# Scan and mixture of experts: logits formed together with the turning back of the rows, rows stored in 4 KB pieces, and another order of work at the end of the first sort

## The reference

```
# scan, for each of 2 sequences of 5056 steps, 256 features
f = lower_bound + (1 - lower_bound) * sigmoid(f_logit);  h = f*h + (1-f)*x;  y[t] = h
# layer 1: 10112 rows, 8 experts, F = 1024
logits = (y/|y|) @ (emb/|emb|).T / tau;  e = argmax(logits)
gate = softmax(logits)[e];  out = gate * (relu(y @ w1[e]) @ w2[e])
# layer 2: the same with logits = out @ w_gate and its own w1, w2
```

## Time and profile before

| | |
|---|---|
| median of 3 runs | 1317.83 us |
| profiled execution | 1315.59 us, span 1313.8 us |
| TensorE busy | 1279.0 us, 97% |
| VectorE busy | 973.1 us, 74% |
| ScalarE busy | 825.5 us, 63% |
| GpSimd busy | 430.6 us, 33% |

### The profile page before, as it was taken

The page is one execution under the profiler, slowest core; times in us unless marked ns, Lnnn a source line. Parts: engine busy times, 40 slices in busy tenths (PEclk is TensorE's granted clock), DMA queues, the critical chain, the costliest instruction groups (busy, mean ns, idle before and its releaser), DMA issues.

```text
span 1313.8 us, 30682 instructions
## 1 busy us (share of the span) xinstructions
PE 1279.0 (97%) x10645; PEld 1243.3 (95%) x10645; DVE 973.1 (74%) x1471; ACT 825.5 (63%) x1390; POOL 430.6 (33%) x460
## 2 busy tenths in 40 slices
PE   7999989999999999999999999999999999999996
PEld 6996579999999999999999999899999999999996
DVE  5887567777777777789877789887777777777772
ACT  5775566666666666666666656666666666666663
POOL 5664121111111111132322153334444444444442
PEclk9998999999999999999999999999999999999998
DMA  7999577676677666769677677567666666766750
GB/s 274 335 322 334 25 244 241 229 231 215 216 228 228 217 219 225 232 211 206 224 227 210 226 205 236 172 198 236 216 225 221 211 231 202 232 219 215 231 168 1
DMA packets 205671, 287.00 MB, mean 218 GB/s; under 512 B 41270, under 2 KB 167876, under 8 KB 205604
## 3 DMA queue, kind: packets, MB, share of 16 engines
q1 hardware_dynamic: 192068, 250.90, 61.5%
q0 software_dynamic: 13536, 35.21, 8.1%
HBM read 252.59 MB, written 35.44 MB: 219 GB/s over the span
## 4 chain that ended last, share of the span: by engine, by line
PE 87%; DVE 6%; issue 3%; ACT 2%; POOL 1%; DMA 0%; SPq 0%; ACTq 0%; DVEq 0%; POOLq 0%
PE bank L1532 38%; PE bank L1512 38%; PE bank L1496 3%; PE bank L1411 2%; PE bank L1376 1%; PE bank L1357 1%; PE bank L1370 1%; DVE hT L454 1%; PE bank L1397 1%; DVE gx L444 1%; ACT w1h L1146 1%; PE bank L1435 1%; POOL fg L1000 1%; DVE tile_oh L581 1%; DVE w1l L421 1%
## 5 line engine op out<-in xcount | busy, mean ns | idle before, releaser
L1512 PE MATMUL bank<-xs,w1h 128*128 128x256 f32 x3008 | 557.1, 283 | 2.9 <-DVE xs L738 1.5
L1512 PEld LDWEIGHTS bank<-xs,w1h 128*128 128x128 f32 x3008 | 459.1, 188 | 3.4 <-DVE xs L738 1.7
L1278 ACT ACTIVATE hh<-bank 128x512 fp32r<-128x512 f32 x376 | 224.9, 598 | 373.1 <-PE bank L1512 331.5
L1532 PE MATMUL bank<-w2h,hl 128*128 128x264 f32 (+1 forms) x1504 | 424.8, 282 | 0.0
L1532 PE MATMUL bank<-w2h,hh 128*128 128x264 f32 (+1 forms) x1504 | 424.8, 282 | 0.0
L1532 PE MATMUL bank<-w2l,hh 128*128 128x264 f32 (+1 forms) x1504 | 424.6, 282 | 0.0
L1512 PE MATMUL bank<-xs,w1l 128*128 128x256 f32 x1504 | 419.9, 279 | 0.0
L749 DVE SCALAR_TENSOR_TENSOR hl<-bank,hh 128x512 fp32r<-128x512 f32 x376 | 259.9, 691 | 174.4 <-ACT hh L1278 170.2
L1532 PEld LDWEIGHTS bank<-w2l,hh 128*128 128x128 f32 x1504 | 283.3, 188 | 0.0
L1532 PEld LDWEIGHTS bank<-w2h,hh 128*128 128x128 f32 x1504 | 283.2, 188 | 0.0
L1532 PEld LDWEIGHTS bank<-w2h,hl 128*128 128x128 f32 x1504 | 282.9, 188 | 0.0
(11 more groups left out here) (173 smaller groups left out, 896.3 us busy)
## 6 DMA issues: line engine op xcount, KB each, us to landing
w1raw<-in_moe_w SPq DMA_DIRECT2D x94, 1024.0 KB
w2raw<-in_moe_w SPq DMA_DIRECT2D x94, 1024.0 KB
rows_b<-yb SPq DMA_DIRECT2D x94, 128.0 KB
xin<-in_x SPq DMA_DIRECT2D x19, 512.0 KB, 5.2
fin<-in_f_logit SPq DMA_DIRECT2D x19, 512.0 KB, 6.7
rows_a<-h_rows SPq DMA_DIRECT2D x19, 512.0 KB, 4.9
w_stage<-in_moe_w SPq DMA_DIRECT2D x12, 512.0 KB, 8.0
xb<-rows_a,row_i POOLq DMA_INDIRECT x94, 4.3
```

The costliest lines, as they stand in the source:

```text
L1278: nc.scalar.activation(hh[:, j, :], bank[j % UB][:, :], ACT.Relu).then_inc(hid_hi, 1)
L1512: ins = mm(bank[j % UB][:, f * GW:(f + 1) * GW], w[p][:, o:o + P], xs[:, p, a, c * GW:(c + 1) * GW], start=k == 0, stop=k == 3 * DC - 1)
L1532: ins = mm(bank[Y_BANK + rows_slot(i, t)][:, 0:n], a[:, j, f * GW + t * P:f * GW + (t + 1) * P], w[p][:, 2 * j + f, 0:n], start=(j, f, k) ...
```

## The change

In the scan, the 8 transposes and the 8 logit products of a chunk become 8 products of `hT` with 136 columns: 128 of the identity and 8 of the embeddings side by side. For the first half of the features the identity stands first, for the second half the embeddings stand first, so that the logits' 8 columns of both halves fall on the same place in the middle and add up there. The result of tile j fills 264 columns of a bank, so banks 4 to 7 are taken as one array `back`. ScalarE copies the rows of all four tiles in one instruction, copies the logits in another (VectorE did it before), and squares. `rows_a` is laid out with partition p's rows behind each other, and `h_rows` has the row's full width of 258 numbers, so that the store of a chunk is one piece of 4128 B per partition. The row number in the table becomes v1 * 79 + v0 instead of v0 * 128 + v1.

At the end of the first sort, the experts are found ahead of the first pair's splits, the splits start two units earlier on ScalarE, `turn_x(0)` comes after `gate_step(14)`, and `up(0, 0)` ahead of `turn_gates`. ScalarE takes `m_x(0)` ahead of `keep_sums(1)` and `m_hidden(0, 0)` ahead of `keep_gates`. The splits of the gate products come behind `m_hidden(0, 1)`.

```diff
-    rows_av = rows_a[1:P * TT + 1, :].rearrange("(t p) w -> p t w", p=P)
+    rows_av = rows_a[TT:(P + 1) * TT, :].rearrange("(p t) w -> p t w", t=TT)
...
+        back = ctx.enter_context(nc.psum_tensor("back", [P, CH, 512], fp32))
+        bank = [ctx.enter_context(nc.psum_tensor(f"bank{n}", [P, 512], fp32)) for n in range(4)]
+        bank += [back[:, n, :] for n in range(CH)]
...
VectorE, start
-            v.tensor_copy(en_T[:, :, :], bank[7][:, 0:DC * E].rearrange("p (c e) -> p c e", c=DC)
+            for c in range(DC):
+                o = (1 - c) * P
+                v.tensor_copy(turn_en[:, c, o:o + E], bank[7][:, c * E:(c + 1) * E]).then_inc(dve_c, 1)
+                v.tensor_copy(turn_en[:, c, c * E:c * E + P], ident[:, :]).then_inc(dve_c, 1)
VectorE, scan
-                    wait(dve, lg_ok, i.value(1, -1))
+                    wait(dve, back_ok, i.value(1, -1))
-                if i.var is not None or i.const > 0:
-                    keep_logits(i.plus(-1), CH)
VectorE, end of the sort
-                link(v.scalar_tensor_tensor(slot_row[:, :], v0, float(P), v1, ALU.mult, ALU.add))
+                link(v.scalar_tensor_tensor(slot_row[:, :], v1, float(TT), v0, ALU.mult, ALU.add))
+                link(v.tensor_scalar(empty[:, :], v1, 0.0, None, ALU.is_equal))
+                mark["table read"] = count[0]
+                find_experts(0, NP)
+                mark["experts"] = count[0]
                 for c in range(DC):
                     split_w1_lo(Index(0), c)
                 for half in range(2):
                     split_w2_lo(Index(0), half)
-                link(v.tensor_scalar(empty[:, :], v1, 0.0, None, ALU.is_equal))
-                find_experts(0, NP)
SyncE
-                sp.dma_start(rows_av[:, bass.ds(k0, nt), 0:D],
-                             h_rows[:, par, 0:nt * D].rearrange("p (t d) -> p t d", d=D)
+                sp.dma_start(rows_av[:, bass.ds(k0, nt), :].rearrange("p t w -> p (t w)"),
+                             h_rows[:, par, 0:nt, :].rearrange("p t w -> p (t w)")
...
+            for b in range(2):
+                sp.wait_ge(h_out[b], 16 * ((NCH + 1 - b) // 2))
             sp.dma_start(rows_av[:, :, D:D + 2], pair[:, 0:TT, :]).then_inc(pair_out, 16)
GpSimd, start
+            const(pool.memset(h_rows[:, :, :, D:ROW], 0.0))
ScalarE, scan
-                    nc.scalar.activation(h_rows[:, par, 2 * b * D:(2 * b + nb) * D],
-                                         bank[4 + b][:, 0:nb * D], ACT.Copy)
+                rows = back[:, 0:nt, 0:DC * (P + E)].rearrange("p t (c x) -> p t c x", c=DC)[:, :, :, 0:P]
+                nc.scalar.activation(h_rows[:, par, 0:nt, 0:D].rearrange("p t (c x) -> p t c x", c=DC), rows,
+                                     ACT.Copy)
+                nc.scalar.activation(logit[:, bass.ds(k.value(CH), nt), :], back[:, 0:nt, P:P + E], ACT.Copy)
ScalarE, end of the sort
-                    if u >= WUNITS - 4:
-                        n = u - (WUNITS - 4)
+                    if u < E + 6:
+                        n = u - (E + 2)
                         (split_w1_hi if n < 2 else split_w2_hi)(Index(0), n % 2)
+                m_x(Index(0))
                 keep_sums(1)
+                m_hidden(Index(0), 0)
                 keep_gates()
TensorE, scan
                 for j in range(nt):
                     for c in range(DC):
-                        o = (j % 2) * D + c * P
-                        ins = nc.tensor.transpose(bank[4 + j // 2][:, o:o + P],
-                                                  hT[:, c, par, j * P:(j + 1) * P], ident[:, :])
+                        ins = mm(back[:, j, c * P:c * P + P + E], hT[:, c, par, j * P:(j + 1) * P], turn_en[:, c, :],
+                                 start=c == 0, stop=c == DC - 1, skip_group_check=True)
                 ins.then_inc(back_ok, 1)
-                wait(pe, lg_kept, k.value())
-                for j in range(nt):
-                    for c in range(DC):
-                        ins = mm(bank[6][:, j * E:(j + 1) * E], hT[:, c, par, j * P:(j + 1) * P],
-                                 en_T[:, c, :], start=c == 0, stop=c == DC - 1)
-                ins.then_inc(lg_ok, 1)
TensorE, end of the sort
                 for u in range(u, WUNITS + 1):
                     gate_step(u)
+                    if u == WUNITS - 2:
+                        pe.wait_ge(dve_c, mark["table read"])
+                        turn_x(Index(0))
+                up(Index(0), 0)
                 turn_gates()
```

More of the change, by code:

```diff
@@ L222, in build @@
         T_BANK, TAB_BANK = [5, 7], 4
-        zrow = yb[0:1, 0, 0:D + 2]
+        zrow = yb[0:TT, 0, 0:D + 2]
         W_BANK = [6, S_BANK]
@@ L371, in build @@
         CHUNK0 = [0, -(-TT // RC), -(-TT // RC) + -(-TA // RC), -(-TT // RC) + -(-TA // RC) + -(-ST // RC)]
-        POOL_CONST = 14
+        POOL_CONST = 15
         LOOP_K = 6
@@ L407, in _ @@
             dve.wait_ge(pe_s, 1)
-            v.tensor_copy(en_T[:, :, :], bank[7][:, 0:DC * E].rearrange("p (c e) -> p c e", c=DC)
-                          ).then_inc(dve_c, 1)
-            count[0] += 1
+            for c in range(DC):
+                o = (1 - c) * P
+                v.tensor_copy(turn_en[:, c, o:o + E], bank[7][:, c * E:(c + 1) * E]).then_inc(dve_c, 1)
+                v.tensor_copy(turn_en[:, c, c * E:c * E + P], ident[:, :]).then_inc(dve_c, 1)
+                count[0] += 2
             for c in range(DC):
@@ L564, in routing @@
                     split_w2_lo(Index(0), half)
-                link(v.tensor_scalar(empty[:, :], v1, 0.0, None, ALU.is_equal))
-                mark["table read"] = count[0]
-                find_experts(0, NP)
-                mark["experts"] = count[0]
             def one_hots(g, t0, w, W):
@@ L780, in step @@
                     m_hidden(i, 1)
+                    if i.var is None and i.const == 0:
+                        split_wg_lo(i)
                     if here(nxt):
@@ L1052, in _ @@
             pool.wait_ge(h_ok, 2 * NCH)
-            pool.wait_ge(lg_ok, NCH)
+            pool.wait_ge(back_ok, NCH)
             number_tables()
@@ L1201, in a_back @@
                 wait(act, h_out[par], k.uses(2, 16))
-                for b in range(2):
-                    nb = min(max(nt - 2 * b, 0), 2)
-                    nc.scalar.activation(h_rows[:, par, 2 * b * D:(2 * b + nb) * D],
-                                         bank[4 + b][:, 0:nb * D], ACT.Copy)
+                rows = back[:, 0:nt, 0:DC * (P + E)].rearrange("p t (c x) -> p t c x", c=DC)[:, :, :, 0:P]
+                nc.scalar.activation(h_rows[:, par, 0:nt, 0:D].rearrange("p t (c x) -> p t c x", c=DC), rows,
+                                     ACT.Copy)
+                nc.scalar.activation(logit[:, bass.ds(k.value(CH), nt), :], back[:, 0:nt, P:P + E], ACT.Copy)
                 for j in range(nt):
-                    o = (j % 2) * D
-                    ins = nc.scalar.activation(sq[:, par, j, :], bank[4 + j // 2][:, o:o + D], ACT.Square,
-                                               accum_out=sumsq[:, bass.ds(k.value(CH, j), 1)])
+                    ins = nc.scalar.activation(sq[:, par, j, :].rearrange("p (c x) -> p c x", c=DC), rows[:, j, :, :],
+                                               ACT.Square, accum_out=sumsq[:, bass.ds(k.value(CH, j), 1)])
                 ins.then_inc(rows_ok, 1)
@@ L1303, in step @@
                 if here(i):
-                    m_hidden(i, 0)
+                    if i.var is not None or i.const > 0:
+                        m_hidden(i, 0)
                     if here(nxt):
@@ L1311, in step @@
                     m_hidden(i, 1)
+                    if i.var is None and i.const == 0:
+                        split_wg_hi(i)
                     if here(nxt):
@@ L1538, in _ @@
             routing()
-            pe.wait_ge(dve_c, mark["table read"])
             tick = beside(resort(0), resort(1))
-            turn_x(Index(0))
             def step(i):
@@ L1545, in step @@
                 first = i.var is None and i.const == 0
-                if here(i):
+                if here(i) and not first:
                     up(i, 0)
```

21 lines of the change are left out of this document (5 added, 16 removed).

## The result

The changed kernel takes 1322.48 us (median of 7 runs, 1321.34 to 1322.80) against 1317.07 us (7 runs, 1315.28 to 1317.95) before: the ratio is 1.004, 95% interval 1.003 to 1.005. The profiled execution took 1322.57 us, 7.0 more than the one of before, and its span is 7.0 longer. The forecast was 7.7 more than the profiled execution, and 1325.5 us for the median.

What follows compares the result with a forecast made beforehand. The prediction took a closed loop of waits between tanhs to bound the scan and TensorE the pairs; 9.6 + 0.5 + 1.2 - 3.6 = +7.7 us gave 1323.3, plus 2.24 for the runs' median 1325.5 us, range 1310 to 1331.

Steps and rivals of the forecast that it cites:

- the ring: Scan: closed loop of waits from one tanh to that two chunks later, 9.49 us, growing 1.07 in 9 turns: +9.6 us.
- the two ways: Scan: paths from the transposes to the tanh, by ScalarE (copies, squares) and by TensorE (logits, next front's first half), ending together.
- Stores: Scan: four 1 KB pieces per partition become one of 4128 B; no engine waits for them, so 0.
- Start: Before the scan: VectorE makes 4 copies in place of 1 ahead of the mark TensorE waits for, +0.5 us.
- Last chunk: Scan's end: the last chunk's turn back runs with the clock down, 12 passes taking 3.0 us; first gate step +1.2 us.
- End of the sort: First sort's end: from the last gate product to `up(0, 3)`, 6.2 us in place of 9.85, so -3.6 us.
- 1: Scan's end: TensorE's clock stays up, 4.0 us less than forecast, 1321.5 us; chance 0.22.
- 2: Scan: the DMA engines set the pace and larger pieces free them, -7.9 us, 1310; chance 0.10.
- 3: Scan: TensorE's way sets the loop between tanhs, so its shortening counts, -8.7 us, 1309; chance 0.10.
- 4: Scan: the loop between tanhs stays as long as it was, -1.9 us, 1316; chance 0.10.
- 5: Sort's end: the gain there is lost to a later wait, 1329 us; chance 0.10.
- 6: Scan: the clock falls since TensorE pauses 1.4 us per chunk, +40 us, 1365; chance 0.05.

Runs made afterwards that it cites:

- e3: Kernel before with only the stores changed to one 4128 B piece per partition, transposes and 8-column products kept; ratio 1.0006 to the kernel before.
- e4: Kernel after with ScalarE's squares moved a chunk later, out of the loop from tanh to tanh; 1308.00 us against 1315.69 for the kernel before.
- e6: Kernel after with the products' end signalled twice, after two tiles and after all; 1310.32 us against 1317.34 for the kernel before.
- e10: Kernel before, unchanged, profiled twice more; the two profiled executions took 1317.41 and 1318.32 us.
- e1: Kernel before with only the new order at the end of the first sort; 1312.71 us against 1315.69 for the kernel before.
- e5: Kernel before with ScalarE's squares moved a chunk later, transposes and 8-column logits kept; ratio 0.9988 to the kernel before, 1.3 us less.
- e9: Kernel before with the logits' products made 128 columns wide in place of 8, the added ones zero; 1323.13 us against 1318.77 for the kernel before.
- e2: Kernel after with the old order at the sort's end, so only the scan's part of the change; 1324.91 us against 1315.69 for the kernel before.
- e7: Kernel after with unused products filling TensorE's pauses around the last chunk's turn back; 1319.82 us, ratio 1.0022 to the kernel before.
- e8: Kernel after with e4 and e6 together, the sort's first steps waiting for the logits' copies only; 1307.58 us against 1317.34 for the kernel before.

## Why the prediction was right, point by point

*What bounds the scan.* Right in the main. That the DMA share of 1.00 is no bound is shown by e3 (share down, time the same). That the kernel after is held by the ring from tanh to tanh and by no engine's load is shown by e4 and e6 (same or more instructions, 12 us less). For the kernel before, TensorE's 97% is not ruled out by them: its way was the one that ended last in the ring (below), and it had 0.18 us of idle time per chunk.

*The ring, forecast +9.6.* From the first tanh (10.03 before, 10.34 after) to the last recurrence's end (105.51 and 114.42) it is +8.6. The 16 passes took 2.12 (forecast 2.1), ScalarE's copy 1.03, the logits' copy less than 0.1 to the next start. The size is off by 1.0 since a turn became 0.95 and not 1.07 longer. The traces show where the 0.12 went. The prediction says that the two ways end together; in fact TensorE's ended last at every turn. Before, the tanh at 72.29 starts 0.04 us after the end of the front's first half, and 0.31 after the start of the last step of the squares; in the kernel after this gap is 0.10:

```profile
71.65 0.60 PE L1357 MATMUL bank<-ident,fin 128*128 128x128 f32 x4
...
71.98 0.24 ACT L1208 ACTIVATION_READ_ACCUMULATOR sq<-bank  x1
```

```profile
67.61 0.24 ACT L1202 ACTIVATION_READ_ACCUMULATOR sq<-back  x1
```

Between 20 and 100 us the gap is 0.21 to 0.39 at all 17 steps before (mean 0.28) and 0.09 or 0.10 at all 16 after. So ScalarE's way had 0.19 us of slack per turn, which the forecast put at nothing, and was lengthened by 1.14 us in the two turns shown (1.03 the passes, 0.08 from their end to the copy, 0.03 from there to the squares); less the slack that is the 0.95 by which the turn grew.

*Stores 0.* Right (e3).

*Start, forecast +0.5.* +0.3 by the first tanh (10.03 to 10.34). In the two executions of e10 the unchanged kernel has it at 9.96 and 10.48, so this is not told from nothing.

*Last chunk, forecast +1.2 with the clock down.* The clock did fall, and it was +1.7. A wait was missed: the last `a_back` waits for the squares of the chunk before, so it began 1.1 us behind the recurrence's end (114.42 to 115.51), not 0.3. Its passes took 2.65, under the 3.0 I had.

*End of the sort, forecast -3.6.* From the first gate step's delay of 10.6 to that of `up(0, 3)` (185.02 against 177.77, 7.25) it is -3.3. In the chain of after `up(0, 1)` and `up(0, 2)` follow without a pause. The second pair's weights were asked for at 163.21, which is 6.6 us before the old time in a kernel that by then ran 10.6 us late: 17 us, as said, and ScalarE did not wait for them:

```profile
163.21 0.39 SPq L832 DMA_DIRECT2D w1raw<-in_moe_w  x1
...
182.19 0.39 SPq L917 DMA_DIRECT2D gates_d<-shifted  x1
...
185.37 0.35 SPq L847 DMA_DIRECT2D wgraw<-gates_d  x1
```

The gate products' way through memory took 3.2 us to the next issue, where it took 8.8 with the weights ahead of it.

*The sum.* 8.6 + 0.3 + 1.7 - 3.3 = 7.3, and 7.0 in the profiled executions; forecast 7.7. That the sum is closer than its terms is luck: 1.0 and 0.2 too much stand against 0.5 and 0.3 too little. In the medians of the runs it is 5.4. The kernel after's median is its profiled execution's time, while before's lies 1.5 above its own: the 2.24 us that the forecast added to get from the one to the other (1323.3 to 1325.5) is the term that failed, since it was a trait of the kernel before and not of both. (The 2.24 also rested on the median of three executions, 1317.83; that of seven is 1317.07.) The profiled execution of before, 1315.59 us, shows no fall of the clock in the scan, while the two of e10, with a clock of 0.98 over 20 to 100 us, took 1317.41 and 1318.32. Of their 1.9 and 2.7 us more in the span, 1.3 and 1.8 lie between the first tanh and the one at 101 to 103 us (90.69 us in the first, 92.00 and 92.49 in e10). The timed executions point the same way: of the 53 of before beside e1, e5 and e9, 17 have a mean granted clock of 0.993 or more over the launch, and their medians lie 1.7, 1.4 and 2.2 us below those of the other 36. So most executions of before have a lower clock, and it goes with about the 1.5 us that are missing; how much of it comes from the scan and how much from the stretch behind is not separated. The same falls stand in e1, e3 and e5, whose `a_back` has the old form. The stretch of 40 to 80 us of e5:

```profile
40.00:80.00 40.00, 38.31 (x311) 37.02 (x311) 30.76 (x43) 29.44 (x95) 23.93 (x24) 0.91 0.97 310
```

Where it fell, one step between tanhs is 5.5 to 5.7 us (e5: 43.97 to 49.46, 64.61 to 70.34), where the same steps of the first profile of before are 4.9 and 5.0. No profile with the 136-column products (after, e2, e4, e6, e7, e8) is under 1.00 there. So the change seems to have bought back a part of what it cost, which the forecast had not seen.

*The rivals.* 1 (clock up at the scan's end) did not come by itself, though e7 shows its mechanism and a price of some 3 us. 2 is ruled out by e3. 3 is half true: before, the tanh really waited for the front, but only by 0.19 us a turn, so that ScalarE's way took over as soon as it grew (e5 against e4). 4 and 5 are ruled out by the period of 5.2 and by e1. 6, a fall of the clock in the scan from TensorE's longer pauses, did not come: it is the form with more busy time whose clock fell.

*A row that was read wrongly.* The prediction doubts the rule on transposes that it cites, because in 8 to 12 us, with nothing but transposes, the granted clock was 1.00. The row says so, but the transposes do not: four of them took 1.06 us there, as in e5 where the clock is 0.50 (48 to 50 us), and 0.60 to 0.63 us at a clock of 1.00 in the scan. In this order: before, e5, and e9, where four took 0.63 at 12.80 us, after transposes alone:

```profile
8.93 1.06 PE L1357 MATMUL bank<-ident,fin 128*128 128x128 f32 x4
```

```profile
49.22 1.06 PE L1367 MATMUL bank<-ident,xin 128*128 128x128 f32 x4
```

```profile
12.80 0.63 PE L1358 MATMUL bank<-ident,xin 128*128 128x128 f32 x4 [0.79 <-issue]
```

By these lengths TensorE ran at half clock in 8 to 12 us, and the row of that stretch is no evidence. The doubt itself holds on other grounds: in e9 the clock had risen with nothing but transposes before it. The forecast took no number from this row.

## What to carry to other kernels

Follow the ring, not the busiest engine. Two ways of nearly equal length between the same two points mean that shortening one is worth nothing and lengthening the other costs its whole length, here 9 us for 1 us in each of 9 turns. Before merging operations that hand over a result, look when the first part of the result could be read: 16 passes that tell their end once cost 12 us more than the same 16 that tell it twice, 7 of them in the ring itself. And work that only follows (the squares) should be placed in the consumer's wait, as long as there is a wait: in e8 the squares themselves are what the copies then stand behind.

## What the runs showed of the hardware

- 16 passes of 128x136 float32 take 2.12 us at full clock, some 0.12 to 0.13 per pass. The weight loads are busy for 1.92 us of the same stretch, so that load and stream overlap, as in the transposes.
- The granted clock fell at the scan's end in before, after, e1, e2, e3, e5 and both of e10, and not in e4, e6, e7, e8 and e9. It fell also between 20 and 100 us in five of the six profiles with transposes and 8-column products (e1, e3, e5, both of e10), with TensorE busy for 38.31 of 40 us in e5. It did not in six kernels with 136-column products, with 35 of 40 in e4 and e8, nor in either of e9. Busy time in the trace does not tell these apart; e9 against e10, with 77.2 and 77.6 of 80 us, is the plainest case.
- The same 128x256 first products took 283 and 279 ns in ten kernels and 285 and 283 in e9, at one clock: a change to another part of a kernel cost 0.8% of the steady stretch without a wait that would show it.
- The row of granted clock shows 1.00 in 8 to 12 us, while four transposes took 1.06 us, their length at 0.50 (e5). The length of a known group tells the clock where the row does not.
- A share of 0.99 of the DMA engines was left at 0.89 by larger pieces with no effect on the time.
